# Gated linear attention with two expert layers: key-row transposes and output products in halves of 32 weight columns

## The chip, the cores and the metric

The kernel runs on one core of a Trainium2 chip. The metric is the device time of one execution in microseconds (us). Three runs of the kernel before gave 957.22, 956.94 and 955.68 us, median 956.94.

## The reference, cut to what matters

```python
# attention: B=4, H=8, S=768, D=48
f = sigmoid(f_logit)
for t in range(S):
    state = f[t][:, None] * state + outer(k[t], v[t])    # one D x D state for each batch and head
    y[t] = q[t] @ state
x = y laid out as [3072, 384]
h = x @ w_in                                    # 384 -> 2048
g = 0 where h <= -1, h where h >= 1, else (h + 1)**2 / 4
x = g @ w_out                                   # 2048 -> 384
x = ((x @ w1) * (x @ w2)) @ w3 @ w_last         # 384 -> 1024 -> 1024 -> 384
```

## The kernel before

The 3072 tokens are eight units of 384. For each unit the first part computes the attention in chunks of 64 tokens and then the first expert layer (`up` and `down`); the second part, from about 610 us on, is the second expert layer. The product w3 @ w_last is made once, at the start (`turn` and `join`). The large products of the expert layers split each fp32 operand into a high and a low part and run three matmuls with 384 moving columns each (`in_parts`, L1075 to L1077 in the first part, L1310 to L1312 in the second).

TensorE's program is one list written out by hand. A round has 32 positions (`ROUND = 2 * T1`); in each stands one `up` or one `down` of the current unit (nine matmuls of 384 columns), and between them small groups of attention work for the next unit, at the positions that tables such as `KROW_AT`, `UPDATE_AT`, `Y_AT` and `X_AT` give. So the matmuls of the experts and the attention groups follow one another on TensorE in an order that doesn't depend on who is ready.

The attention groups on TensorE, for one unit of six chunks, four pairs of heads (`PAIRS = 4`), D = 48:

- `k`, `q`, `tot`, `leaf`: transposes of whole tiles into columns (L975, L982, L987, L992).
- `level` n = 0 to 3 (L1013): scores between the two halves of blocks. `keys` is 64 weight columns at n = 0 to 2 and 32 weight columns at n = 3; the moving operand has 32 columns. 48 matmuls each.
- `krow` n = 0, 1 (L1024): the keys of three chunks turned back into rows with the identity as moving operand: 64 weight columns, 48 moving columns, 24 matmuls.
- `update` n = 0, 1 (L1037): key rows times values: 48 weight columns, 48 moving columns, 24 matmuls (16 in the last group of every second unit).
- `y` n = 0 to 2 (L1050 `within`, L1056 `carried`): the output rows of two chunks, scores times values plus queries times state: 64 weight columns, 48 moving columns, 32 matmuls.
- `x` n = 0 to 2 (L1070): the output rows turned into columns.

All of `level`, `krow`, `update` and `y` use quarters of the array: 64 rows of it by 64 columns (the row half from the partitions that the operands start at, the column half from the partitions of the output in PSUM). Four such matmuls after one another go to four different quarters; `corners(i)` gives the order for `level`, `krow` and `update`, `turns` for `y`. All operands of these groups are plain fp32, and every such matmul stands in the trace as two weight loads and two matmul records. So a `krow` has 48 records, a `y` 64, an `update` 48 (or 32), a `level` 96. The whole transposes have one record each.

A group starts by waiting for its inputs and for the bank pair `wide` that it writes, and its last matmul releases ScalarE (L609 for `krow`, L616 for `y`), which copies the result out.

Of the kernel before, what the change touches and what calls it, by code (L numbers as in the profile page):

```python
# [33 lines left out]
CHUNK = 64  # L34
# [58 lines left out]
def first_part(nc, given):  # L93
# [8 lines left out]
    B, H, S, D, DM, F1, UNIT, UNITS = (given[n] for n in "B H S D DM F1 UNIT UNITS".split())  # L102
    PT, PAIRS, CHUNKS, KD, T1, TT, BLOCK = (given[n] for n in "PT PAIRS CHUNKS KD T1 TT BLOCK".split())
    LEAFROW = LEAF * D
    R = HEAD_ROWS + D
    HALF, LEVELS = CHUNK // 2, len(BLOCK)
    G = 3
    y_acc, h_bank, att_bank = banks[0:3], banks[3:5], banks[5:8]
    wide = given["small_banks"][:, 0:2]

    with ExitStack() as ctx:
# [5 lines left out]
        ident = place("ident", [P, P])  # L117
# [7 lines left out]
        kw = place("k_cols", [R, PAIRS, UNIT])  # L125
        qd = place("q_cols", [R, PAIRS, UNIT])
# [3 lines left out]
        scores = place("scores", [P, PAIRS, CHUNKS, CHUNK])  # L130
# [236 lines left out]
        def head_rows(ab):  # L367

            return slice(HEAD_ROWS * ab, HEAD_ROWS * ab + D)
# [9 lines left out]
        def score_half(ab, pair):  # L379

            return half_rows(ab ^ (pair // 2))

        def half_rows(n):

            return slice(CHUNK * (n % 2), CHUNK * (n % 2 + 1))
# [577 lines left out]
        def _(pe):  # L963
            def corners(i):

                return (0, i), (1, i), (0, i + PAIRS // 2), (1, i + PAIRS // 2)

            def attention(grp, u):
                kind, n = grp[0], grp[-1]
                bank = bank_of(u, grp)  # L970
                wait_bank(pe, u, grp)
                if kind == "tot":
                    wait(pe, "prefix", u, 3)
                    for pair in range(PAIRS):
                        last = nc.tensor.transpose(bank[0:R, pair * PT:(pair + 1) * PT], padded_pair(fn, pair, 3),  # L975
                                                   ident[0:PT, 0:PT])
                    last.then_inc(sems["tot_tr"], 1)
                elif kind == "k":
                    wait(pe, "carry", u, 3)
                    wait(pe, "k_in", u, 16 * LEAF)  # L980
                    for j in range(LEAF):
                        last = nc.tensor.transpose(bank[0:R, j * PT:(j + 1) * PT], padded_pair(kn, n, j), ident[0:PT, 0:PT])  # L982
                    last.then_inc(sems["k_tr"], 1)
                elif kind == "q":
                    wait(pe, "query4", u, 4)
                    for j in range(LEAF):
                        last = nc.tensor.transpose(bank[0:R, j * PT:(j + 1) * PT], padded_pair(qn, n, j), ident[0:PT, 0:PT])  # L987
                    last.then_inc(sems["q_tr"], 1)
                elif kind == "leaf":
                    wait(pe, "leaf_add", u, 3)  # L990
                    for j in range(LEAF):
                        last = nc.tensor.transpose(bank[:, j * PT:(j + 1) * PT],  # L992
                                                   yl[:, j].rearrange("p h d -> p (h d)")[:, n * P:(n + 1) * P],
                                                   ident[0:PT, 0:PT])
                    last.then_inc(sems["leaf_tr"], 1)
                elif kind == "level":
                    c = BLOCK[n]
                    if n == 0:
                        wait(pe, "q_ev", u, PAIRS)
                        wait(pe, "k_ev", u, PAIRS)  # L1000
                    else:
                        wait(pe, "q_next", u, n)
                        wait(pe, "k_next", u, n)
                    for m in range(CHUNKS):
                        at_ = m * CHUNK
                        for i in range(PAIRS // 2):
                            for ab, pair in corners(i):
                                o = (pair % 2 * CHUNKS + m) * HALF
                                later_half = qd[head_rows(ab), pair, at_:at_ + CHUNK]\
                                    .rearrange("p (b h c) -> p b h c", h=2, c=c)[:, :, 1]  # L1010
                                keys = HALF if n == LEVELS - 1 else CHUNK
                                to = score_half(ab, pair).start
                                last = nc.tensor.matmul(wide[to:to + keys, pair // 2, o:o + HALF],  # L1013
                                                        kw[head_rows(ab), pair, at_:at_ + keys], later_half,
                                                        start=True, stop=True)
                    last.then_inc(sems["level_mm"], 1)
                elif kind == "krow":
                    wait(pe, "k_next", u, LEVELS)
                    for c in range(G):
                        at_ = (G * n + c) * CHUNK  # L1020
                        for i in range(PAIRS // 2):
                            o = (c * PAIRS // 2 + i) * D
                            for ab, pair in corners(i):
                                last = nc.tensor.matmul(wide[score_half(ab, pair), pair // 2, o:o + D],  # L1024
                                                        kw[head_rows(ab), pair, at_:at_ + CHUNK],
                                                        ident[head_rows(ab), head_rows(ab)], start=True, stop=True)
                    last.then_inc(sems["krow_tr"], 1)
                elif kind == "update":
                    wait(pe, "krow_ev", u, n + 1)
                    wait(pe, "vb_in", u, per_unit["vb_in"])  # L1030
                    for c in range(G):
                        if G * n + c == CHUNKS - 1 and u % 2:
                            break
                        for i in range(PAIRS // 2):
                            o = (c * PAIRS // 2 + i) * D
                            for ab, pair in corners(i):
                                last = nc.tensor.matmul(wide[head_rows(ab), pair // 2, o:o + D],  # L1037
                                                        krow[score_half(ab, pair), n, pair // 2, o:o + D],
                                                        vb[score_half(ab, pair), G * n + c, pair, :], start=True, stop=True)
                    last.then_inc(sems["update_mm"], 1)  # L1040
                elif kind == "y":
                    wait(pe, "masked", u, 2 * LEVELS)
                    wait(pe, "q_next", u, LEVELS)
                    wait(pe, "state_new", u, (2 * n + 1) * PAIRS)

                    def within(r, c, pair, stop):

                        m = 2 * n + c
                        o = (pair if pair < PAIRS // 2 else pair + PAIRS // 2) * D
                        return nc.tensor.matmul(wide[half_rows(c), r, o:o + D], scores[half_rows(r), pair, m, :],  # L1050
                                                vb[half_rows(r), m, pair, :], start=True, stop=stop)

                    def carried(r, c, pair, start):

                        m, o = 2 * n + c, pair * D
                        return nc.tensor.matmul(wide[half_rows(c), r, o:o + D], qd[head_rows(r), pair, m * CHUNK:(m + 1) * CHUNK],  # L1056
                                                state[head_rows(r), state_at(m), pair, :], start=start, stop=True)

                    turns = [(r, r ^ c) for c in range(2) for r in range(2)]
                    for pair in range(PAIRS):  # L1060
                        for r, c in turns:
                            last = within(r, c, pair, pair >= PAIRS // 2)
                        for r, c in turns:
                            last = carried(r, c, pair, pair >= PAIRS // 2)
                    last.then_inc(sems["y_mm"], 1)
                elif kind == "x":
                    wait(pe, "y_ev", u, n + 1)
                    wait(pe, "y_add", u, 2 * n + 2)
                    for d in range(KD):
                        last = nc.tensor.transpose(bank[:, d * P:(d + 1) * P], yn[:, d * P:(d + 1) * P], ident[:])  # L1070
                    last.then_inc(sems["x_tr"], 1)
# [305 lines left out]
```

## Time and profile before

| | us |
|---|---|
| median of three runs | 956.94 |
| the profiled execution: its own time | 958.38 |
| its span, first to last instruction | 956.4 |
| TensorE matmuls busy (PE) | 911.5 |
| TensorE weight loads busy (PEld) | 882.3 |
| VectorE busy (DVE) | 530.8 |
| ScalarE busy (ACT) | 398.5 |

The span is what the profile's views cover; the 2.0 us between 958.38 and 956.4 lie around it. A record's duration includes its way through the array, so that records overlap: the pace of a group is read from starts, not from durations. In an answer in order of time, a row merges neighbouring records of one kind; the start of the next row is when the next kind starts. Column PEclk is the granted clock of TensorE: 1.00 is 2.4 GHz, 0.50 is 1.2 GHz.

### The profile page before, as it was taken

To read this page: it belongs to the slowest core of one execution; us is meant where nothing else is said; L and a number is where in the kernel's file an instruction comes from. 1 tells how busy PE (TensorE), PEld (TensorE's weight loads), DVE (VectorE), ACT (ScalarE), POOL (GpSimd) and SP (SyncE) were. 2 spreads that over 40 slices of the span, in tenths; PEclk is the share of its full clock that TensorE was granted. 3 is DMA by queue.
4 is the path that set the end of the run, shared out by engine and by line. 5 is a ranking of instruction groups with operands and counts; after the bars stand their busy time and mean duration, and the time that the engine had idled before them with its cause. 6 is when DMAs were issued, how large, how long until landed. Compare 5 with 4: busy or idle time off the path is not lost.

```text
span 956.4 us, 24664 instructions
## 1 busy us (share of the span) xinstructions
PE 911.5 (95%) x10824; PEld 882.3 (92%) x10824; DVE 530.8 (56%) x993; ACT 398.5 (42%) x805; POOL 148.0 (15%) x151
## 2 busy tenths in 40 slices
PE   0679799999999999999999999999999999999998
PEld 0669699999999999999999999999999999999998
DVE  6655688866867767767767764464222222222322
ACT  1322365555544644645544544574222232222222
POOL 2320503403403404305205100000000000000000
PEclk9968899999999999999999999999999999999999
DMA  9940570160160260250430200512011011010000
GB/s 270 234 111 27 173 110 3 26 127 2 27 126 2 51 102 2 64 89 2 84 69 2 51 3 1 207 42 75 1 50 50 1 50 50 1 51 25 1 25 25
DMA packets 112554, 57.69 MB, mean 60 GB/s; under 512 B 92480, under 2 KB 108096, under 8 KB 111936
## 3 DMA queue, kind: packets, MB, share of 16 engines
q1 hardware_dynamic: 112448, 56.11, 24.5%
q8 instruction: 86, 1.41, 0.6%
q14 instruction: 20, 0.16, 0.1%
HBM read 45.09 MB, written 11.01 MB: 59 GB/s over the span
## 4 chain that ended last, share of the span: by engine, by line
PE 92%; DVE 5%; DMA 1%; ACT 1%; issue 1%; SPq 0%; DVEq 0%; ACTq 0%
PE bank L1075 17%; PE bank L1077 15%; PE bank L1076 15%; PE bank L1312 10%; PE bank L1311 10%; PE bank L1310 10%; PE bank L1013 5%; PE bank L1024 2%; PE bank L1050 2%; PE bank L1056 1%; PE bank L1037 1%; PE bank L982 1%; PE bank L987 1%; DMA first_q<-in_q_dram 1%; PE bank L992 1%; PE bank L1070 1%
## 5 line engine op out<-in xcount | busy, mean ns | idle before, releaser
L1280 DVE TENSOR_TENSOR product<-bank,a_copy 128x384 f32<-128x384 f32 x64 | 35.7, 557 | 219.1 <-PE bank L1312 219.1
L1075 PE MATMUL bank<-x_hi,w_in_hi 128*128 128x384 f32 x384 | 135.5, 353 | 0.5 <-DVE x_lo L896 0.5
L1075 PE MATMUL bank<-g_hi,w_out_hi 128*128 128x384 f32 x384 | 133.6, 348 | 0.3 <-DVE g_lo L907 0.3
L1077 PE MATMUL bank<-x_hi,w_in_lo 128*128 128x384 f32 x384 | 129.3, 337 | 0.0
L1076 PE MATMUL bank<-x_lo,w_in_hi 128*128 128x384 f32 x384 | 129.2, 336 | 0.0
L1077 PE MATMUL bank<-g_hi,w_out_lo 128*128 128x384 f32 x384 | 128.7, 335 | 0.0
L1076 PE MATMUL bank<-g_lo,w_out_hi 128*128 128x384 f32 x384 | 128.6, 335 | 0.0
L1312 PE MATMUL bank<-y_hi,w_lo 128*128 128x384 f32 x384 | 128.3, 334 | 0.0
L1310 PE MATMUL bank<-y_hi,w_hi 128*128 128x384 f32 x384 | 128.3, 334 | 0.0
L1311 PE MATMUL bank<-y_lo,w_hi 128*128 128x384 f32 x384 | 128.3, 334 | 0.0
L653 ACT ACTIVATE g_hi<-gated 128x384 fp32r<-128x384 f32 x128 | 67.2, 525 | 128.1 <-DVE gated L902 128.0
L1234 ACT ACTIVATE a_copy<-bank 128x384 f32<-128x384 f32 x64 | 31.5, 492 | 183.4 <-PE bank L1312 183.4
L902 DVE SCALAR_TENSOR_TENSOR gated<-bank,gated 128x384 f32<-128x384 f32 x128 | 70.8, 553 | 59.8 <-ACT gated L647 59.7
L644 ACT ACTIVATE gated<-bank 128x384 f32<-128x384 f32 x128 | 62.4, 488 | 99.2 <-PE bank L1077 99.2
L907 DVE TENSOR_TENSOR g_lo<-gated,g_hi 128x384 fp32r<-128x384 f32 x128 | 71.5, 559 | 21.9 <-ACT g_hi L653 21.9
L1075 PEld LDWEIGHTS bank<-x_hi,w_in_hi 128*128 128x128 f32 x384 | 72.5, 189 | 2.8 <-DVE w_out_lo L390 0.6
L1075 PEld LDWEIGHTS bank<-g_hi,w_out_hi 128*128 128x128 f32 x384 | 72.0, 188 | 2.7 <-DVE g_lo L907 0.9
L530 POOL TENSOR_TENSOR y_leaf<-q_leaf,k_leaf 96x384 f32<-96x384 f32 x28 | 34.0, 1242 | 259.3 <-PE bank L992 259.3
L1076 PEld LDWEIGHTS bank<-x_lo,w_in_hi 128*128 128x128 f32 x384 | 72.7, 189 | 0.0
L1077 PEld LDWEIGHTS bank<-x_hi,w_in_lo 128*128 128x128 f32 x384 | 72.5, 189 | 0.0
L1076 PEld LDWEIGHTS bank<-g_lo,w_out_hi 128*128 128x128 f32 x384 | 72.2, 188 | 0.0
L1077 PEld LDWEIGHTS bank<-g_hi,w_out_lo 128*128 128x128 f32 x384 | 72.1, 188 | 0.0
(113 smaller groups left out, 1759.9 us busy)
## 6 DMA issues: line engine op xcount, KB each, us to landing
v_leaf<-in_v_dram SPq DMA_DIRECT2D x8, 576.0 KB, 6.5
v_rows<-in_v_dram SPq DMA_DIRECT2D x64, 72.0 KB, 2.8
middle<-middle_out SPq DMA_DIRECT2D x8, 576.0 KB, 2.8
w_rows<-in_moe_w_dram SPq DMA_DIRECT2D x8, 512.0 KB, 10.4
f_leaf<-in_f_logit_dram SPq DMA_DIRECT2D x28, 144.0 KB, 3.9
k_leaf<-in_k_dram SPq DMA_DIRECT2D x28, 144.0 KB, 4.7
q_leaf<-in_q_dram SPq DMA_DIRECT2D x28, 144.0 KB, 4.2
out_dram<-out_rows SPq DMA_DIRECT2D x7, 576.0 KB, 3.3
```

The lines of the kernel that those rows point to most:

```text
L644: nc.scalar.activation(gt[:, i % RING], h_bank[i % 2][:, 0:UNIT], ACT.Relu, bias=0.5, scale=0.5)\
L653: nc.scalar.activation(g[0][:, i % RING], gt[:, i % RING], ACT.Copy).then_inc(sems["g_hi"], 1)
L902: nc.vector.scalar_tensor_tensor(gt[:, i % RING], h_bank[i % 2][:, 0:UNIT], 1.0, gt[:, i % RING], ALU.max, ALU.min).then_inc(sems["gated"], 1)
L907: nc.vector.tensor_tensor(g[1][:, i % RING], gt[:, i % RING], g[0][:, i % RING].bitcast(F32), ALU.subtract)\
L1013: last = nc.tensor.matmul(wide[to:to + keys, pair // 2, o:o + HALF], kw[head_rows(ab), pair, at_:at_ + keys], later_half, start=True, stop ...
L1075: nc.tensor.matmul(o, w[0], b[0], start=first, stop=False)
L1076: nc.tensor.matmul(o, w[0], b[1], start=False, stop=False)
L1077: return nc.tensor.matmul(o, w[1], b[0], start=False, stop=last_)
L1280: nc.vector.tensor_tensor(pf[:, f % RING], b_bank[f % 2][:, 0:UNIT], af[:, f % 2], ALU.mult)\
L1310: nc.tensor.matmul(o, w[0], b[0], start=first, stop=False)
L1311: nc.tensor.matmul(o, w[0], b[1], start=False, stop=False)
L1312: return nc.tensor.matmul(o, w[1], b[0], start=False, stop=last_)
```

## The change

Each matmul of `krow` and of `y` becomes two, with 32 weight columns each: the first and the second 32 positions of the chunk (krow) or of the queries (y), going to the first and the second 32 partitions of the output half that the whole matmul wrote. The moving operand stays 48 columns wide and is now streamed twice. The order within four matmuls is as before, with the first parts of four matmuls and then their second parts. `level` and `update` are untouched, and so are all waits, releases and positions in the list.

```diff
-                            for ab, pair in corners(i):
-                                last = nc.tensor.matmul(wide[score_half(ab, pair), pair // 2, o:o + D],
-                                                        kw[head_rows(ab), pair, at_:at_ + CHUNK],
-                                                        ident[head_rows(ab), head_rows(ab)], start=True, stop=True)
+                            for part in range(2):
+                                for ab, pair in corners(i):
+                                    to = score_half(ab, pair).start + part * HALF
+                                    last = nc.tensor.matmul(wide[to:to + HALF, pair // 2, o:o + D],
+                                                            kw[head_rows(ab), pair, at_ + part * HALF:at_ + (part + 1) * HALF],
+                                                            ident[head_rows(ab), head_rows(ab)], start=True, stop=True)
...
-                    def within(r, c, pair, stop):
+                    def queries(c, part):
+                        at_ = CHUNK * (c % 2) + HALF * part
+                        return slice(at_, at_ + HALF)
+
+                    def within(r, c, part, pair, stop):
...
-                        return nc.tensor.matmul(wide[half_rows(c), r, o:o + D], scores[half_rows(r), pair, m, :],
+                        return nc.tensor.matmul(wide[queries(c, part), r, o:o + D],
+                                                scores[half_rows(r), pair, m, part * HALF:(part + 1) * HALF],
                                                 vb[half_rows(r), m, pair, :], start=True, stop=stop)
-                    def carried(r, c, pair, start):
+                    def carried(r, c, part, pair, start):
                         m, o = 2 * n + c, pair * D
-                        return nc.tensor.matmul(wide[half_rows(c), r, o:o + D], qd[head_rows(r), pair, m * CHUNK:(m + 1) * CHUNK],
+                        at_ = m * CHUNK + part * HALF
+                        return nc.tensor.matmul(wide[queries(c, part), r, o:o + D], qd[head_rows(r), pair, at_:at_ + HALF],
                                                 state[head_rows(r), state_at(m), pair, :], start=start, stop=True)
-                    turns = [(r, r ^ c) for c in range(2) for r in range(2)]
+                    turns = [(r, r ^ c, part) for part in range(2) for c in range(2) for r in range(2)]
                     for pair in range(PAIRS):
-                        for r, c in turns:
-                            last = within(r, c, pair, pair >= PAIRS // 2)
-                        for r, c in turns:
-                            last = carried(r, c, pair, pair >= PAIRS // 2)
+                        for r, c, part in turns:
+                            last = within(r, c, part, pair, pair >= PAIRS // 2)
+                        for r, c, part in turns:
+                            last = carried(r, c, part, pair, pair >= PAIRS // 2)
```

## Rows read from the trace of the kernel before

**Rows 1.** The page: busy time, clock by slices, chain by engine.

```profile
PE 911.5 (95%) x10824; PEld 882.3 (92%) x10824; DVE 530.8 (56%) x993; ACT 398.5 (42%) x805; POOL 148.0 (15%) x151
PEclk9968899999999999999999999999999999999999
PE 92%; DVE 5%; DMA 1%; ACT 1%; issue 1%; SPq 0%; DVEq 0%; ACTq 0%
```

**Rows 2.** Busy time by stretch: from:to, length, busy of each engine (records), clock.

```profile
60.00:130.00 70.00, 60.28 (x839) 55.99 (x840) 43.51 (x73) 25.63 (x47) 16.65 (x16) 0.81 0.39 93
130.00:600.00 470.00, 469.38 (x7537) 447.20 (x7537) 340.54 (x676) 238.33 (x485) 114.20 (x102) 1.00 0.24 45
```

**Rows 3.** Groups of matmuls by form: line, rows*weight columns, out<-moving, records | busy, mean ns.

```profile
L1050 PE MATMUL bank<-v_rows,scores 64*64 64x48 f32 x768 | 24.8, 222 | 2.2 <-DVE state L875 2.2
L1056 PE MATMUL bank<-state,q_cols 48*64 48x48 f32 x768 | 24.0, 218 | 0.0
L1024 PE MATMUL bank<-ident,k_cols 48*64 48x48 f32 x768 | 15.9, 232 | 0.0
L1037 PE MATMUL bank<-v_rows,k_rows 64*48 64x48 f32 x704 | 11.4, 208 | 1.4 <-DVE y_rows L883 1.4
L1013 PE MATMUL bank<-q_cols,k_cols 48*32 48x32 f32 x768 | 8.7, 201 | 6.5 <-DVE q_cols L815 6.5
```

**Rows 4.** TensorE in order of time, one y group: start, length, row of records.

```profile
309.87 0.33 PE L1050 MATMUL bank<-v_rows,scores 64*64 64x48 f32 x8
...
310.72 0.30 PE L1056 MATMUL bank<-state,q_cols 48*64 48x48 f32 x8
310.95 0.44 PE L1075 MATMUL bank<-x_hi,w_in_hi 128*128 128x384 f32 x1
```

**Rows 5.** The same view, one krow group.

```profile
306.93 0.92 PE L1024 MATMUL bank<-ident,k_cols 48*64 48x48 f32 x48
307.78 0.45 PE L1075 MATMUL bank<-g_hi,w_out_hi 128*128 128x384 f32 x1
```

**Rows 6.** The same view: a level group with 64, then one with 32 weight columns.

```profile
274.64 1.60 PE L1013 MATMUL bank<-q_cols,k_cols 48*64 48x32 f32 x96
276.17 0.45 PE L1075 MATMUL bank<-x_hi,w_in_hi 128*128 128x384 f32 x1
...
286.61 1.02 PE L1013 MATMUL bank<-q_cols,k_cols 48*32 48x32 f32 x96
287.56 0.44 PE L1075 MATMUL bank<-g_hi,w_out_hi 128*128 128x384 f32 x1
```

**Rows 7.** The same view: update groups of 48 and of 32 records.

```profile
295.39 0.76 PE L1037 MATMUL bank<-v_rows,k_rows 64*48 64x48 f32 x48
296.08 0.45 PE L1075 MATMUL bank<-g_hi,w_out_hi 128*128 128x384 f32 x1
...
314.62 0.58 PE L1037 MATMUL bank<-v_rows,k_rows 64*48 64x48 f32 x32
315.13 0.44 PE L1075 MATMUL bank<-x_hi,w_in_hi 128*128 128x384 f32 x1
```

**Rows 8.** L1013 alone, windows from the 32-column group's start: length, busy (records so far).

```profile
286.60:286.63 0.03, 0.02 (x4) 1.00 0.00 0
286.60:287.00 0.40, 0.39 (x44) 1.00 0.00 0
286.60:287.40 0.80, 0.79 (x92) 1.00 0.00 0
```

**Rows 9.** L1050 alone, windows from the y group's start.

```profile
309.86:309.90 0.04, 0.03 (x4) 1.00 0.00 0
309.86:309.96 0.10, 0.09 (x4) 1.00 0.00 0
309.86:310.00 0.14, 0.13 (x8) 1.00 0.00 0
```

**Rows 10.** TensorE in order of time at half clock, 32-column level, then krow.

```profile
64.11 1.51 PE L1013 MATMUL bank<-q_cols,k_cols 48*32 48x32 f32 x96 [6.46 <-DVE q_cols L815]
65.54 0.69 PE L1075 MATMUL bank<-w_last_hi,w_turned_hi 128*128 128x384 f32 x1
...
67.78 1.53 PE L1024 MATMUL bank<-ident,k_cols 48*64 48x48 f32 x48
69.24 0.69 PE L1075 MATMUL bank<-w_last_hi,w_turned_hi 128*128 128x384 f32 x1
```

**Rows 11.** Who waited for whom from 130 to 600 us, TensorE and its readers.

```profile
PEld bank L1050 <- issue: 3.2, 15, 0.2
PEld bank L1024 <- issue: 1.7, 7, 0.3
ACT y_rows L616 <- PE bank L1056: 1.9, 1, 1.9
ACT k_rows L609 <- PE bank L1024: 1.2, 6, 0.2
```

## The prediction

> **What bounds the kernel now.** I read the page first. TensorE's matmuls are busy for 95% of the span and the chain that ended last runs over TensorE for 92% of it [rows 1]. The busy share alone doesn't say that TensorE is the bound at the place of the change, so I next read the windows: from 130 to 600 us, where seven of the eight units' attention stands between the first expert layer's products, TensorE is busy for 469.38 of 470.00 us at granted clock 1.00 [rows 2]. Nothing there is waiting that a longer group could eat into. Before that, from 60 to 130 us, it is 60.28 of 70.00 us at a mean clock of 0.81 [rows 2]: this is the first unit, where some of TensorE's time is idle. The order of TensorE's work is a fixed list, so in the full stretch a nanosecond more or less in a group is one in the span. The question is only whether 32 weight columns at twice the count run faster or slower than 64.
>
> **What the change adds.** krow has 768 records and y 768 + 768 in all [rows 3]; each count doubles. Nothing moves, no wait is added, and the switches to and from quarters of the array stay one per group. The duration of a record (218 to 232 ns) says nothing here, since they overlap deeply; what counts is the time from a group's first start to the next kind's first start:
>
> - y, 64 records of 64 weight columns: 309.87 to 310.95, 1.08 us [rows 4]. There are 24 such groups.
> - krow, 48 records of 64 columns: 306.93 to 307.78, 0.85 us [rows 5]. There are 16, and two of them at half clock.
> - level, 96 records of 64 columns, 32 moving: 274.64 to 276.17, 1.53 us; the last level, 96 records of 32 columns: 286.61 to 287.56, 0.95 us [rows 6].
> - update, 48 records of 48 columns: 295.39 to 296.08, 0.69 us; 32 records: 314.62 to 315.13, 0.51 us [rows 7].
>
> From these I take out a fixed part and a pace. y less krow is 0.23 us for 16 records: 14.4 ns a record at 64 columns; fixed part 0.85 - 48 x 0.0144 = 0.16 us. Update: 0.18 us for 16 records, 11.3 ns at 48 columns, fixed 0.15 us. The last level with fixed 0.15: 0.80 / 96 = 8.3 ns at 32 columns. The level with 64 columns: 1.38 / 96 = 14.4 ns, though its moving operand is 32 wide and y's is 48. So in these rows the pace follows the weight columns, 14.4, 11.3, 8.3, and the moving width doesn't show.
>
> **Why halving the columns doesn't halve the pace.** A line through the three is 0.19 ns per column plus 2.2 ns. Two records of 32 columns cost 16.6 ns where one of 64 costs 14.4. Two further views say where the 2.2 ns sit. In y, four records start within 0.04 us, none more within 0.10, and the next four by 0.14 [rows 9]: the array takes four and then makes the fifth wait, and this fifth goes to another quarter than the first (if the two records of a matmul follow one another, four records are two matmuls, one per row half). The wait is then not for the same quarter to come free but for something that the column halves of a row half share; by the pace, the loading of weights. If it is that, eight tiles in place of four change nothing: the columns to be loaded per row half are the same. In the 32-column level, four records start within 0.03 us, but from 0.40 to 0.80 us 48 records start, 92 - 44, one each 8.3 ns [rows 8]. Here the supply of instructions may be what is short; that too would not get better with more of them.
>
> **The sum.** The new matmuls have just the form of the last level's: 48 (or 64) rows, 32 weight columns, in the same order over row and column halves. I take its pace, since it is the only row with 32 columns, and its fixed part.
>
> - y: 0.15 + 128 x 0.0083 = 1.21 us against 1.08: +0.13. Times 24: +3.1 us.
> - krow at full clock: 96 records, exactly the count of the last level: 0.95 against 0.85, +0.10. Times 14: +1.4 us.
> - krow at half clock, two: now 67.78 to 69.24, 1.46 us for 48 records; the last level of that unit, 96 records of 32 columns at half clock, takes 64.11 to 65.54, 1.43 us [rows 10]. At this clock two halves cost what one whole costs: 0.
>
> Sum +4.5 us. Three y groups stand in the first unit, where a wait behind them could take up their 0.13; that is 0.4 us at most and I leave it in. The evacuations behind the groups wait for them: ScalarE waited in this stretch 1.2 us for krow and 1.9 us for y in all [rows 11], and its copy and the next group that needs it keep their distance in the list, so they move along with it. The idle of the weight loads put down to issue, 3.2 us over 15 y groups and 1.7 over 7 krow groups [rows 11], is about 0.2 us per group, the switch to quarters; its count doesn't change.
>
> The span goes from 956.4 to 960.9 us and the profiled execution's own time from 958.38 to 962.9. That execution is 1.4 us above the median, 0.15%. On the median the forecast is 956.94 + 4.5 = **961.4 us**.
>
> Bounds of the unknown pace, since no row has eight tiles in turn with 48 moving columns. From above, the update's 11.3 ns, the nearest row whose moving operand is 48 wide and whose weights are not wider than it. From below, the spacing within four, 0.02 to 0.03 us for three intervals, that is 7 to 8 ns; read at its fastest, 6.7 ns [rows 8]. The pace at which nothing changes is (1.08 - 0.15) / 128 = 7.3 ns for y and 0.70 / 96 = 7.3 for krow.
>
> **A rule to weigh.** The Trainium skill, page TensorEngine Tiling, section Performance Considerations, puts an overhead of about 60 cycles on each matmul and advises against tiling along a dimension that is already small. At 2.4 GHz that would be an estimated 25 ns per record, y would go to some 3.3 us and krow to 2.5, and the sum to about +80 us. The rows contradict the size (8.3 ns per record at 32 columns) and agree with the direction: a part that doesn't shrink with the columns is paid twice.
>
> **The rivals.**
>
> *Streaming becomes the bound.* Every row so far has moving columns no more than weight columns. With 32 weight columns and 48 moving ones, the 48 may set the pace: then a record costs what it does in update, where both are 48, 11.3 ns. y: 0.15 + 128 x 0.0113 = 1.60, +0.52, times 24 is +12.4; krow 1.23, +0.38, times 14 is +5.4; the two at half clock some 0.4 us each, with 11.3 ns raised as the 32-column pace is from full to half clock (8.3 to 1.28 / 96 = 13.3 ns [rows 10]). Some +19 us, 976 us. For it: the update can't tell 48 weights from 48 moving. Against it: 64-column groups with 32 and with 48 moving have one pace. Decides above 8.3 ns as soon as streams of one row half exclude each other.
>
> *The eight tiles do overlap: faster.* If the fifth record waits for its own part of the array and a column group of 32 is free of it, the pace is that of records within a four, 6.7 ns. y: 0.15 + 128 x 0.0067 = 1.01, -0.07, times 24 is -1.7; krow 0.79, -0.06, times 14 is -0.8; at half clock krow would fall from 1.46 to about 0.8 at best, -1.3 for two. Sum -3.8 us, 953.1 us. It decides once the pace is below 7.3 ns. For it: four starts in 0.03 us. Against it: the last level has quarters to spare in the same way and holds 8.3 ns over half of its length. Further still: the two halves side by side at the cost of one, y 0.15 + 64 x 0.0083 = 0.68, krow 0.55; -9.6 and -4.2, 943 us.
>
> The Trainium skill's page TensorEngine Tiling, section Tiling Modes, has eight tiles in a 64 x 32 configuration and lets different tiles load weights and multiply in parallel. By this rule that further case would be the result; the start of the fifth record in y, over 0.05 us after the fourth though it goes to another tile, speaks against it.
>
> *Between the two.* The 32-column pace is nearer 7.3 to 7.7 ns for some groups (their first records are faster than their last), or the first unit hides its part: within 0.2% of before, 1.9 us, which is about what a measurement of this kernel can tell from no change.
>
> **How the numbers follow.** The forecast, a pace between 7.9 and 9 ns: chance 0.66, with a range of its own of 959 to 965 us. Streaming or another loss per record up to 11.3 ns: 0.13. Within 1.9 us: 0.10. Faster: 0.11, of which 0.03 is the further case. The range leaves out the faster cases and the top of the streaming one: 957 to 971. Chances: faster 0.11, within 0.12 (with a little of the forecast's lower end), slower 0.77.
>
> **What the changed profile would show.** y from first start to the next kind's at 1.21 us and krow at 0.95; 48 records of either in 0.40 us in the later part of a group; TensorE still busy for all but 1 us between 130 and 600 us, with that work ending about 4 us later; level and update unchanged at 1.53, 0.95 and 0.69 us; the krow pair at half clock still 1.46 us. I'm wrong by the first rival if y takes 1.6 us, and by the second if it takes about 1.0 us or less. If the groups grow as said and the time doesn't, the cover in the first unit, or a change of the granted clock there, is where to look.

## The result, and the profile after

The changed kernel took 980.67 us (median of four, 976.88 to 983.44) against 957.08 us before: ratio 1.0248, 95% interval 1.0223 to 1.0273. It is 23.6 us slower, where 4.5 us were forecast; the time lies above the range.

The profiled execution took 976.88 us with a span of 974.9 us, 18.5 us more than the span before. TensorE's time by stretch, where 470 us had 469.38 busy before [rows 2]:

```profile
130.00:600.00 470.00, 462.25 (x9166) 439.91 (x9159) 338.58 (x654) 234.11 (x474) 111.60 (x102) 1.00 0.24 46
```

The stretch that was full now has 7.75 us idle. Who waited for whom there, on TensorE:

```profile
PE bank L1065 <- issue: 3.9, 3, 2.1
PE bank L1057 <- issue: 2.0, 2, 1.8
PE bank L1084 <- DVE g_lo L907: 1.4, 2, 1.0
PE bank L1013 <- DVE k_cols L834: 0.3, 1, 0.3
```

L1057 and L1065 are the two matmul lines of y now. "issue" means that nothing the profile shows held the engine: five gaps of 5.9 us in all, inside y groups. Before, the same view put none down to issue. One more of 5.3 us stands in the first unit:

```profile
PE bank L1057 <- issue: 5.3, 1, 5.3
```

In order of time, the end of the first y of the third unit:

```profile
237.61 0.20 PE L1065 MATMUL bank<-state,q_cols 48*32 48x48 f32 x1
239.94 0.31 PE L1065 MATMUL bank<-state,q_cols 48*32 48x48 f32 x14 [2.13 <-issue]
240.19 0.45 PE L1084 MATMUL bank<-g_hi,w_out_hi 128*128 128x384 f32 x1
```

The group stops 14 records before its end, for 2.3 us between starts, with all its inputs there (a group waits only at its head). That's one part of the loss. The other is seen in groups without such a gap, a y and a krow, to be laid beside [rows 4] and [rows 5]:

```profile
309.45 0.31 PE L1057 MATMUL bank<-v_rows,scores 64*32 64x48 f32 x15
...
310.76 0.44 PE L1084 MATMUL bank<-g_hi,w_out_hi 128*128 128x384 f32 x1
...
302.65 1.09 PE L1026 MATMUL bank<-ident,k_cols 48*32 48x48 f32 x96
303.67 0.44 PE L1084 MATMUL bank<-x_hi,w_in_hi 128*128 128x384 f32 x1
```

y takes 1.31 us (before 1.08), krow 1.02 us (before 0.85). How a krow runs inside shows in windows from its start, L1026 alone (length, busy, records so far), as in [rows 8]:

```profile
302.64:302.86 0.22, 0.21 (x32) 1.00 0.35 74
302.64:302.90 0.26, 0.25 (x32) 1.00 0.30 63
302.64:302.94 0.30, 0.29 (x33) 1.00 0.26 55
302.64:303.14 0.50, 0.49 (x54) 1.00 0.16 33
302.64:303.34 0.70, 0.69 (x75) 1.00 0.11 23
```

32 records start within 0.22 us, under 7 ns apart on the mean. Then a pause of nearly 0.1 us, and from there 21 records per 0.20 us, 9.5 ns each. 32 records with their 32 weight loads are 64 instructions. The page's row for instruction transfers (packets, MB, share of time), before and after, went from 86 to 104 packets:

```profile
q8 instruction: 86, 1.41, 0.6%
q8 instruction: 104, 1.70, 0.7%
```

18 packets more for 2304 more matmul records and as many weight loads, 4608 instructions: 256 instructions per packet, and 1.70 MB / 104 is 16.3 KB. Around the gap shown above, the transfers of the core in 40 slices from 236 to 241 us:

```profile
GB/s 0 0 0 0 0 0 0 0 131 0 0 0 0 0 0 0 0 0 0 0 0 0 0 0 0 0 0 0 0 0 0 0 0 0 0 0 0 0 0 131
DMA packets 2, 0.03 MB, mean 7 GB/s; under 512 B 0, under 2 KB 0, under 8 KB 0
```

Nothing else was moved: one such packet in the slice at 237.0 us and the next in the slice at 240.9, 3.9 us apart, and in between TensorE resumed at 239.94. So the theory after the result had two parts. *Queue:* some 64 instructions lie ready at a group's start and run at the array's pace; after them the array waits for instructions, at 4.2 to 4.7 ns each. *Blocks:* instructions arrive in blocks of 256, one per 3.5 to 4 us at best; a y of 256 instructions uses up a block in 1.2 us, and where the boundaries lie badly the next isn't there. The rival: the 48-wide stream sets the pace (the prediction's first rival), and the gaps have to do with the groups themselves.

### The profile page after: what moved, and what is told of

The parts are those of the page before. It is cut to its first block, busy times and chain, and to the rows that moved or that the text cites. A ratio compares the mean times of both kernels' runs of the same rounds, so it can differ in the third digit from the quotient of the medians.

```text
span 974.9 us, 29272 instructions
## 1 busy us (share of the span) xinstructions
PE 918.1 (94%) x13128; PEld 887.2 (91%) x13128; DVE 534.6 (55%) x993; ACT 400.3 (41%) x805; POOL 145.4 (15%) x151
## 4 chain that ended last, share of the span: by engine, by line
PE 91%; DVE 5%; issue 2%; DMA 1%; ACT 1%; SPq 0%; DVEq 0%; ACTq 0%
PE bank L1084 16%; PE bank L1086 14%; PE bank L1085 14%; PE bank L1321 10%; PE bank L1319 10%; PE bank L1320 10%; PE bank L1013 4%; PE bank L1057 2%; PE bank L1026 2%; PE bank L1065 1%; PE bank L1039 1%; PE bank L987 1%; PE bank L982 1%; PE bank L992 1%; DMA first_q<-in_q_dram 1%
## 5 line engine op out<-in xcount | busy, mean ns | idle before, releaser
L907 DVE TENSOR_TENSOR g_lo<-gated,g_hi 128x384 fp32r<-128x384 f32 x128 | 75.0, 586 | 21.9 <-ACT g_hi L653 21.9
```

What stands on the lines that cost most here:

```text
L907: nc.vector.tensor_tensor(g[1][:, i % RING], gt[:, i % RING], g[0][:, i % RING].bitcast(F32), ALU.subtract)\
```

## The experiments

Medians and ratios are against the kernel before on the same chip.

**krow alone in halves.** The krow part of the diff, y as before.

> Only krow in halves; y as before. Supply theory (the array takes 32 records of 32 weight columns in 0.2 us, then the engine waits for instructions, which come at about 4.2 ns each, and in blocks of 256 that are fetched one ahead): krow 1.02 us from its first start to the next kind's as in the changed kernel, against 0.85, so 14 x 0.17 = +2.4 us, less about 0.5 in the two groups at half clock, and few long gaps: 958 to 961 us. Streaming theory (48 moving columns set the pace): the same krow. If instead the long gaps come with any added instructions, about a third of the 23 us: 963 to 967 us.

958.51 us, ratio 1.0021 (1.0010 to 1.0032), 1.8 us more than 956.73 and in the range given. krow takes 1.02 us, and one gap of 0.5 us is put down to issue between 130 and 620 us. These added instructions don't bring long gaps.

**y alone in halves.**

> Only y in halves; krow as before. Supply theory: y 1.31 us where undisturbed against 1.08, 24 x 0.23 = +5.5 us, and gaps of 1 to 2 us inside some y groups, since one y group is 256 instructions, a whole block: 968 to 978 us. Streaming theory: +5.5 us and no long gaps, 962 to 964 us.

968.25 us, ratio 1.0119 (1.0099 to 1.0138), +11.5 us, at the low end of the range given. About 5.5 of it are 24 groups at 0.23. From 130 to 620 us:

```profile
PE bank L1082 <- issue: 1.8, 1, 1.8
PE bank L1082 <- DVE gated L902: 1.2, 1, 1.2
```

The gap of 1.8 us now stands right behind a y, at the first large matmul (L1082). It cost more than itself; two windows, the gap and what follows:

```profile
162.00:165.00 3.00, 1.83 (x9) 1.83 (x10) 2.05 (x4) 0.52 (x1) 3.00 (x4) 0.93 0.02 5
165.00:168.00 3.00, 3.00 (x11) 3.00 (x11) 0.00 (x0) 0.00 (x0) 0.33 (x1) 0.50 0.00 0
```

After the gap, the granted clock falls to 0.50, 1.2 GHz, and in these 3 us the large matmuls start 0.32 us apart where they start 0.174 us apart at 1.00. Such a fall doesn't follow every gap: in the changed kernel's own profile the clock is 1.00 from 130 to 600 us in spite of its gaps. Its other runs left no trace, only a lower mean clock: 976.88 us at 0.984, 983.44 at 0.977. A mean lower by 0.007 over 980 us is an estimated 6.9 us of work lost, and the two times differ by 6.6. The krow and y results add up to 13 us, not 23.6. By the block theory that is no contradiction: how many instructions stand ahead of a group differs in all three kernels, and so does where the gaps fall.

**As many instructions, split the other way.** Each matmul of krow and y is split along its moving columns; the weights stay 64 wide.

```diff
-    last = nc.tensor.matmul(wide[score_half(ab, pair), pair // 2, o:o + D],
-                            kw[head_rows(ab), pair, at_:at_ + CHUNK],
-                            ident[head_rows(ab), head_rows(ab)], start=True, stop=True)
+    at, one = o + part * D // 2, HEAD_ROWS * ab + part * D // 2        # part: 0, 1
+    last = nc.tensor.matmul(wide[score_half(ab, pair), pair // 2, at:at + D // 2],
+                            kw[head_rows(ab), pair, at_:at_ + CHUNK],
+                            ident[head_rows(ab), one:one + D // 2], start=True, stop=True)
...                                                                    # y likewise
```

> The same number of instructions as the changed kernel, but each matmul of krow and y split along its moving columns, 24 and 24, with 64 weight columns in both. Weight-load theory: 14.4 ns per record whatever streams, so y 0.15 + 128 x 0.0144 = 2.0 us, krow 1.53; 24 x 0.92 + 14 x 0.68 + 2.4 = +34 us, and shorter gaps because a block lasts longer: 988 to 996 us. Streaming theory: records with 24 moving columns are no slower than with 48, y at most 1.3 us, 970 to 980 us.

993.78 us, ratio 1.0397, in the range of the theory by weight loads and 14 us above the other's. A y and a krow:

```profile
252.10 0.31 PE L1053 MATMUL bank<-v_rows,scores 64*64 64x24 f32 x8
...
254.10 0.44 PE L1080 MATMUL bank<-x_hi,w_in_hi 128*128 128x384 f32 x1
...
155.99 1.59 PE L1027 MATMUL bank<-ident,k_cols 48*64 48x24 f32 x96
157.51 0.45 PE L1080 MATMUL bank<-x_hi,w_in_hi 128*128 128x384 f32 x1
```

2.00 and 1.52 us, as from 14.4 ns per record. With half the stream a record of 64 weight columns costs what it did with the whole: the weight columns set the pace there, not the stream. The gaps stay: in this trace and in the changed kernel's, y groups are interrupted behind the same three records counted from the program's start (the 2228th, 3615th and 6393rd matmul). The two kernels share the count of instructions and the list around the groups; the shape and the order of the matmuls in a y differ. The gaps are shorter here, 1.4 to 1.6 us between starts in place of 1.8 to 2.3.

**Waits as filler.** The kernel before, with instructions in y that only wait for a semaphore long reached:

```diff
                         for r, c in turns:
                             last = within(r, c, pair, pair >= PAIRS // 2)
+                            met_waits(pe)      # eight waits on constants, four instructions in the program
```

> The kernel before with y and krow whole, and in each y group 124 added instructions that only wait for a semaphore that is long there, four after each matmul: as many instructions as the changed y has, no added work for the array. Supply theory: eight instructions per matmul, 33 ns, where the array needs 29: y about 1.2 to 1.3 us, and the long gaps inside y come too: 966 to 976 us. Streaming or array theory: the waits cost nothing or a few ns, no long gaps: 957 to 959 us.

1298.37 us, ratio 1.356. Neither theory. TensorE in order of time inside a y:

```profile
340.87 0.28 PE L1060 MATMUL bank<-state,q_cols 48*64 48x48 f32 x2 [0.29 <-issue]
341.31 0.28 PE L1060 MATMUL bank<-state,q_cols 48*64 48x48 f32 x2 [0.16 <-issue]
341.75 0.28 PE L1054 MATMUL bank<-v_rows,scores 64*64 64x48 f32 x2 [0.16 <-issue]
```

One matmul (two records) per 0.44 us in place of 0.029: each of the four wait instructions, though met, cost about 0.1 us. It is no cheap filler, and the run says nothing on blocks. It does show that the two records of a matmul follow one another.

**The boundaries moved.** Nothing is changed but the head of TensorE's program, where met waits are put in front, by 128, by 256 and by 64 instructions (two waits make one instruction):

```diff
-            pe.wait_ge(constants, CONSTANTS)
+            for _ in range(257):               # 513 and 129 in the other two
+                pe.wait_ge(constants, CONSTANTS)
```

> The changed kernel with 128 instructions more at the head of TensorE's program (waits that are met), so that each boundary between blocks of 256 instructions falls 128 instructions earlier in the work. Supply theory: krow 1.02 and undisturbed y 1.31 as before, but the gaps of over 1 us stand in other groups, at places that again lie a multiple of 256 instructions apart; total anywhere from 966 to 988 us. If the gaps belong to the groups themselves (their data, their position in the list), they stay in the first y group of the second, third and fifth unit.

963.49 us, ratio 1.0080 (1.0065 to 1.0095): +8.2 us. The same work with 128 instructions more is 17 us faster than the changed kernel, 15.4 us if each is taken against the kernel before on its own chip. The range given started at 966 us: I had expected the long gaps to stand elsewhere, and they are gone. All of TensorE's waits from 130 to 620 us, and its busy time:

```profile
PE bank L1013 <- DVE k_cols L834: 0.3, 1, 0.3
PE bank L1084 <- DVE x_lo L896: 0.2, 1, 0.2
...
130.00:590.00 460.00, 459.66 (x9191) 1.00 0.24 45
```

Not one gap is put down to issue. 23 of the 24 y groups take 1.30 to 1.31 us, and one 1.39. In the changed kernel 12 take that, and the other 12 are 0.2 to 6.0 us longer, 15.2 us in all, so half of them had lost time, most of them too little to show as a wait.

> The changed kernel with 256 instructions more at the head of TensorE's program, so that the boundaries between blocks of 256 fall at the same places in the work as without any. Block theory: the long gaps are back in the first y group of the second, third and fifth unit, near its 110th record, and after the third y of the second unit; 976 to 984 us. If the added waits at the head had helped in another way (a later start, less crowded transfers), it would stay near the 963.5 us of the shift by 128.

989.92 us, ratio 1.0338. The end of the same y as above:

```profile
246.79 0.20 PE L1065 MATMUL bank<-state,q_cols 48*32 48x48 f32 x1
248.85 0.41 PE L1065 MATMUL bank<-state,q_cols 48*32 48x48 f32 x14 [1.85 <-issue]
249.19 0.69 PE L1084 MATMUL bank<-g_hi,w_out_hi 128*128 128x384 f32 x1
```

Again 14 records before its end (and here the granted clock fell behind the gap: the large matmul takes 0.69 us in place of 0.45), and likewise the gaps in the second and fifth unit and in the first. The place was forecast, the time wasn't: the whole program stands some 9 us later (246.79 against 237.61), which the 256 waits at the head took (the 193rd matmul starts 9.6 us later already, and in the shift by 128 it starts 0.8 us earlier than in the changed kernel); less them it is about the changed kernel's time. The group is the same in all three kernels; only the count of instructions ahead of it, modulo 256, decides.

The traces say the same once more, by a count of all that stands in them for TensorE, waits included. In the changed kernel 2753, 4545, 5569, 7361 and 12993 instructions start before the five gaps of 1 us and more that the shift by 128 doesn't have. All five numbers leave 193 when divided by 256. The third of these gaps, 1.0 us, is the longer of the two that the view put down to DVE g_lo, and it belongs here too. In the shift by 256 each number is 256 higher. In the kernel with y alone in halves they are 4289 (the gap of 1.8 us) and 7361 (the one of 1.2 us that was put down to DVE), in the one with the moving columns split 4545, 7361 and 12993. The single gaps of 0.5 us with krow alone in halves and in the shift by 64 leave 193 too. And the packets fit. Put them beside the boundaries in order, the first packet beside the 449th instruction, the second beside the 705th and so on: in none of the traces does TensorE start the first instruction behind a boundary less than about 1.2 us after the end of its packet, and behind the five gaps it starts 1.35 to 1.5 us after. In the changed kernel 16 boundaries come within 1.6 us of their packet, in the shift by 128 two, in the kernel before none. That is what shows that TensorE waits for its instructions there.

> The same with 64 instructions more: the boundary that stood 220 to 230 instructions into a first y group stands some 160 in. Block theory: a block then spans about 4.3 us of work in place of 3.8, where the gap came to 2 us; gaps of at most 1.5 us at about the 80th record or at another group; 963 to 977 us, between the other two.

967.07 us, ratio 1.0098 (1.0072 to 1.0124): +8.7 us. One gap of 0.5 us from 130 to 620 us, so the long ones of that stretch are gone at 64 already. That is within the range given, but no gap came at the 80th record. How near a boundary may lie isn't settled by this.

**y in four parts.** Between two parts of y stand three of the large matmuls that follow, so that instructions can queue up. Once in halves (32 records a part), once whole (16 records), krow whole in both:

```diff
-                    for pair in range(PAIRS):
-                        for r, c, part in turns:
-                            last = within(r, c, part, pair, pair >= PAIRS // 2)
...
+                    one_pair(0)
+                    held_back.extend((one_pair, pair) for pair in range(1, PAIRS))
...
                 for kk in range(KD):                    # in up, and likewise in down
...
+                    next_part()                         # one pair of y after three large matmuls
```

> y in halves but in four parts of 32 records, with three of the following large matmuls between two parts; krow as before. Supply theory: each part is served from the queue: 0.20 us from first to last start and 0.13 to the next, about 0.33; each part costs 0.43 us over the large matmuls around it with the switch there and back, y 1.71 in place of 1.17, +13 us, and no long gaps: 968 to 972 us. Streaming theory: 9.2 ns per record also in a part, 0.43 us per part, +23 us: 980 us.

> The kernel before with y in four parts of 16 records (64 weight columns), three large matmuls between two parts. Both theories: 0.21 us from first to last start and 0.15 to the next, 0.36 us a part, 0.03 us longer than a part in halves; y +0.64 us, +15 us: 971 to 974 us. Against parts_half, supply theory: slower by 24 x 4 x 0.03 = 2.9 us. Streaming theory: faster than parts_half by 7 us or more.

987.49 us (ratio 1.0333) in halves, 989.50 us (1.0352) whole. The first part of a y, in halves and then whole:

```profile
163.43 0.31 PE L1062 MATMUL bank<-v_rows,scores 64*32 64x48 f32 x15
...
163.76 0.44 PE L1093 MATMUL bank<-g_hi,w_out_hi 128*128 128x384 f32 x1
```

```profile
163.48 0.33 PE L1057 MATMUL bank<-v_rows,scores 64*64 64x48 f32 x8
...
163.85 0.45 PE L1086 MATMUL bank<-g_hi,w_out_hi 128*128 128x384 f32 x1
```

0.33 us against 0.37 us for the same work, and the version in halves is the faster one as a whole too: 987.34 to 987.90 us against 988.05 to 990.76 (medians 2.0 us apart, where the supply theory gave 2.9 and the streaming theory 7 the other way). With 0.13 us of it behind the last start, a part in halves has its 32 records in 0.20 us, 6.5 ns each at 48 moving columns. That refutes the streaming rival, which needed 9.2, and shows that halves are the faster form for the array as long as their instructions are there. The totals came out 15 to 19 us above what I had expected: the later y_mm makes TensorE wait, in the version in halves with

```profile
PE bank L1088 <- DVE y_rows L883: 7.4, 6, 1.2
```

(1.2 us in each of six units; 6.9 us in the whole version), which I had left out. The rest of the excess isn't accounted for.

**Whole and halves mixed in one y.** One pair of the four in halves, the first or the last; krow whole.

```diff
-                    turns = [(r, r ^ c, part) for part in range(2) for c in range(2) for r in range(2)]
                     for pair in range(PAIRS):
+                        turns = [(r, r ^ c, part) for part in (range(2) if pair == 0 else (None,))
+                                 for c in range(2) for r in range(2)]   # None: 64 columns; PAIRS - 1 in the other
```

> krow as before; in y only the first of four pairs in halves (32 records), the other three whole (48 records): 80 records. Supply theory: the first 32 take 0.20 us in place of 0.23, but empty the queue, after which some 0.1 us pass; then 14.4 ns a record. With a switch of array form inside the group that may cost up to 0.1 more: y 1.10 to 1.25 against 1.08, 957.5 to 961 us, no long gaps. Streaming theory: 32 x 9.2 in place of 16 x 14.4, +0.06 us, 958.5 us.

> krow as before; in y the first three pairs whole (48 records) and the last in halves (32 records). If the 0.13 us after the 32nd record of the earlier mixed y came from an emptied queue, then here, where the group ends with the halves, there is none, and y is 0.03 to 0.05 us shorter than before: 24 x -0.04 = -1 us, 954.5 us. If it came from the change of array form inside a group, it comes here too, after the 48th record: y 0.1 us longer, +2 to +3 us, 958 us.

959.05 us, ratio 1.0039 (1.0026 to 1.0051), and 960.96 us, ratio 1.0035 (1.0018 to 1.0051): +3.8 and +2.6 us against the kernel before on their chips. The version with the halves last:

```profile
229.83 0.33 PE L1055 MATMUL bank<-v_rows,scores 64*64 64x48 f32 x8
...
230.45 0.30 PE L1062 MATMUL bank<-state,q_cols 48*64 48x48 f32 x8
230.68 0.31 PE L1055 MATMUL bank<-v_rows,scores 64*32 64x48 f32 x15
...
231.01 0.44 PE L1081 MATMUL bank<-g_hi,w_out_hi 128*128 128x384 f32 x1
```

Eight records before took 0.12 us from row to row; the eight at 230.45 are followed only after 0.23. So going from 64 to 32 weight columns inside a group costs about 0.11 us, in the order in which the queue should not be empty (48 records of 64 columns use 7.2 ns per instruction, more than the 4.2 to 4.7 of the supply). y takes 1.18 us, 0.10 more than before. The 0.11 us is more than the 0.04 us that a pair in halves saves. Neither mix beats the kernel before.

## Why the prediction was wrong

**The bound.** Right: TensorE is the bound, and in the stretch after the first unit each added nanosecond arrived in the time. The shift by 128 gives it nearly undisturbed: 24 x 0.23 + 14 x 0.17 = 7.9 us from the groups' lengths, and 8.2 us measured.

**The pace.** A size that was off. The forecast took 0.15 us + 8.3 ns per record from the last level, y 1.21 and krow 0.95; it measured 1.31 and 1.02, so this term of the sum was 7.9 and not 4.5 us. The last level's average hid two things that happen to have nearly one pace. In its trace the 5th to the 36th record start 8.2 ns apart, and the later ones 8.5, with no pause between. By the queue theory the first come from the queue and only the later ones at the rate at which instructions are supplied, which the prediction named for it. In halves over eight tiles the first 32 records start in 0.2 us, then nothing starts for 0.1 us, and the rest of 96 or 128 records comes at about 9.4 ns, not 8.3. No run varied that rate by itself: that it is the supply is argued, and where the extra 1 ns per record comes from stays open.

**What shares the load.** Wrong. The step "if it is that, eight tiles in place of four change nothing" does not stand: 32 records run at 6.5 ns each over eight tiles, where the 64-column form needs two times 7.2 ns for the same pair of halves, and where the last level, 32 weight columns over four tiles, needs 8.2. The second rival's pace, 6.7 ns, is what the array does. It doesn't last past the queue, which is why the rival's sum never came.

**Streaming.** The first rival gave 976 us, the nearest of the forecasts to 980.67, for a cause that isn't there: y took 1.31 us and not 1.6, and the parts in halves run at 6.5 ns with 48 moving columns.

**The missing term.** The step that failed for most of the 23.6 us is "each count doubles ... nothing moves, no wait is added". A count of instructions was taken as a count of work for the array. It is a load on another resource too, their delivery in blocks of 256, which the sum had at nothing. In the profiled execution the gaps put down to issue sum to 11.2 us (5.3 + 3.9 + 2.0), with 1.4 us of waits put down to DVE, of the 14.2 us between its span and the 960.7 us of the shift by 128. Laid side by side by the number of the matmul, the changed kernel falls behind the other by 5.6, 1.8, 1.1, 2.3 and 2.0 us at the five gaps, 12.8 us. The difference of the medians, 17 us, is larger; the lower mean clock of the other three runs fits that, but none of them has a trace. The page before gave the two numbers that this needed: 86 packets for instructions, and 1.41 MB. A y would have come out at one whole block in 1.2 us, and in the trace before no two of those packets start less than 4.0 us apart after 130 us, a first sign of what a block may take.

The Trainium skill, page Runtime: NRT & Kernel Launch, section Instruction fetch mechanics, has 16 KiB blocks of 256 instructions, fetched while the current one runs. It also says that fetching stays hidden because the sequencer dispatches more slowly than blocks arrive. The block size agrees with the page's packets here. The second doesn't hold in this kernel: TensorE took instructions at 4.2 to 4.7 ns each, a block in about 1.2 us, and fetches stood 3.9 us apart. The measurement decides. The Trainium skill, page Advanced Engine Details and Errata, section Engine Queue Depths, gives TensorE a queue of 64; the 32 records and 32 weight loads before the pause agree.

**What the prediction asked the changed profile.** TensorE busy for all but 1 us between 130 and 600: no, 7.75 us idle. 48 records of either in 0.40 us in the later part of a group: no, 42. level and update unchanged: yes where no gap falls. The krow pair at half clock: one of the two, 66.30 to 67.62 us, took 1.32 us against 1.46 [rows 10], so at this clock it was shorter in halves and not equal, and the other ran at full clock this time.

## What to carry to other kernels

Splitting a matmul for the array's sake pays only while its instructions are in the queue: count the instructions of a burst, not only its columns, and compare with 64. Then count instructions per microsecond over some hundreds: here a burst of 256 in 1.2 us met a fetch of one block per 3.3 us at best in any run and mostly 3.5 to 4 around the gaps, and whether it stalled depended on where the block boundary fell. Where such a kernel's time jumps after an edit far away, add instructions at the head to move the boundaries before looking for another cause.

## What the runs showed of the hardware that I had not expected

- 128 instructions in front of the same program changed its time by 17 us (980.67 to 963.49), and 256 brought the gaps back at the same records. The gaps of 1 us and more that come and go with these shifts all stand at one remainder, 193, of the count of TensorE's instructions divided by 256.
- A wait instruction that is long met cost TensorE about 0.1 us between small matmuls (0.44 us per matmul with four of them behind it, against 0.029).
- Going from 64 to 32 weight columns within the tiled form cost about 0.11 us.
- After a gap of 1.8 us in a busy stretch, the granted clock stood at 0.50 for the 3 us from 165 to 168, and matmuls started 0.32 us apart in place of 0.174. A gap can so cost nearly twice itself (an estimate: 1.4 us of work lost in these 3 us, beside the 1.8).
